# Attention scores of the 64-query step: two 64x64 matmuls, or one over the whole array with diagonal query blocks

## What is computed

```python
# attention: batch 4, heads 12, sequence 448, head dimension 64, all float32
scores = scale * q @ k.T                 # scale = 1/sqrt(64)
scores = cap * tanh(scores / cap)        # cap = 30
scores = scores - max(scores, axis=-1)
attn = exp(scores); attn = attn / (sum(attn, axis=-1) + 1e-9)
x = attn @ v                             # -> (1792, 768)
# first MLP: y = relu(x @ w_in)**2 @ w_out        (d_ff 2048)
# second: a greedy router gives each of 8 experts 224 tokens, then relu(y_e @ w1[e]) @ w2[e]
```

## Time and profile before

| | us |
|---|---|
| median of 3 runs | 1107.17 (1106.67 to 1107.28) |
| the profiled execution, its own time | 1108.04 |
| its span, first to last instruction | 1106.3 |
| attention, up to the first matmul of the MLP | 0 to 333.6 of the span |
| TensorE busy over the span | 1042.9 |
| VectorE busy | 828.0 |
| ScalarE busy | 599.2 |

### The profile page before, as it was taken

One profiled execution on the slowest core, in us unless ns is written; L12 is line 12 of the kernel. 1 busy time (PEld: TensorE's weight loads), 2 busy tenths in 40 slices (PEclk: granted clock), 3 DMA queues, 4 the chain that ended last, 5 costly groups with the idle time before them and its releaser, 6 DMA issues.

```text
span 1106.3 us, 24810 instructions
## 1 busy us (share of the span) xinstructions
PE 1042.9 (94%) x9468; PEld 846.1 (76%) x9468; DVE 828.0 (75%) x1678; ACT 599.2 (54%) x948; POOL 201.2 (18%) x322
## 2 busy tenths in 40 slices
PE   4999999899989999999999999999995999999996
PEld 1444444444449899999999999999994988888885
DVE  2989998999995965666586665566667899999971
ACT  3877777888865433323362111111326688777881
POOL 1534443444340000000000000000002132122201
PEclk9999999999999999999999999999996999999999
DMA  3561111212006000000150000002265566777401
GB/s 78 164 182 50 50 58 43 59 50 66 18 17 229 1 3 1 2 1 1 31 200 24 4 27 27 26 27 100 67 229 168 181 259 256 274 276 266 164 14 50
DMA packets 56996, 103.53 MB, mean 94 GB/s; under 512 B 6224, under 2 KB 34640, under 8 KB 56912
## 3 DMA queue, kind: packets, MB, share of 16 engines
q1 hardware_dynamic: 54352, 91.33, 24.4%
q0 software_dynamic: 2560, 11.01, 3.3%
HBM read 91.32 MB, written 11.01 MB: 93 GB/s over the span
## 4 chain that ended last, share of the span: by engine, by line
PE 83%; DVE 6%; issue 4%; ACT 4%; DMA 1%; POOL 1%; ACTq 1%; SPq 0%; DVEq 0%; POOLq 0%
PE psum L1516 20%; PE psum L1449 20%; PE psum L1650 10%; PE psum L1636 9%; PE psum L1387 6%; PE psum L1398 6%; PE psum L1407 4%; PE psum L1565 2%; DVE arena L950 2%; PE psum L1418 1%; ACT arena L652 1%; PE psum L1536 1%; PE psum L1618 1%; PE psum L1460 1%; ACT arena L647 1%
## 5 line engine op out<-in xcount | busy, mean ns | idle before, releaser
L1516 PE MATMUL psum<-arena 128*128 128x224 f16 x2304 | 232.3, 259 | 0.0
L1449 PE MATMUL psum<-arena 128*128 128x224 f16 x2304 | 223.7, 259 | 0.0
L1449 PEld LDWEIGHTS psum<-arena 128*128 128x128 f16 x2304 | 220.0, 98 | 2.9 <-issue 1.5
L1516 PEld LDWEIGHTS psum<-arena 128*128 128x128 f16 x2304 | 215.8, 98 | 1.0 <-issue 0.2
L525 POOL TENSOR_SCALAR arena<-arena 128x448 f32<-128x448 f32 x168 | 107.8, 652 | 178.8 <-DVE arena L932 178.7
L1650 PE MATMUL psum<-arena 128*112 128x384 f16 x768 | 127.1, 326 | 0.4 <-issue 0.4
L652 ACT ACTIVATE arena<-arena 128x448 f32<-128x448 f32 x168 | 125.7, 750 | 0.3 <-DVE arena L952 0.3
L1407 PEld LDWEIGHTS psum<-arena 128*112 128x112 f32 x672 | 71.7, 135 | 67.4 <-issue 53.3
L641 ACT ACTIVATE arena<-psum,arena 128x896 f32<-128x896 f32 x96 | 87.8, 914 | 63.9 <-PE psum L1387 63.6
L1650 PEld LDWEIGHTS psum<-arena 128*112 128x112 f16 x768 | 99.3, 130 | 24.8 <-issue 0.8
L1636 PE MATMUL psum<-arena 128*128 128x224 f16 x1152 | 114.5, 262 | 3.5 <-DVE arena L1300 2.0
(11 more groups left out here) (222 smaller groups left out, 1304.9 us busy)
## 6 DMA issues: line engine op xcount, KB each, us to landing
arena<-moe_w SPq DMA_DIRECT2D x16, 3072.0 KB, 12.4
arena<-moe_w_out SPq DMA_DIRECT2D x32, 384.0 KB, 3.8
arena<-moe_w_in SPq DMA_DIRECT2D x16, 384.0 KB, 5.4
arena<-q SPq DMA_DIRECT2D x24, 224.0 KB, 2.9
arena<-k SPq DMA_DIRECT2D x24, 224.0 KB, 3.1
arena<-v SPq DMA_DIRECT2D x24, 224.0 KB, 2.6
y_rows<-arena SPq DMA_DIRECT2D x16, 336.0 KB, 3.2
arena<-y_rows,arena POOLq DMA_INDIRECT x16, 4.5
```

Of the source, the lines that this page charges most:

```text
L1449: last = pe.matmul(out, w_split[:, f, z, k * 128:(k + 1) * 128], x[u % 2][:, k, :], start=(k == 0 and m == 0), stop=(k == KD - 1 and m == 2))
L1516: last = pe.matmul(out, w_split[:, k, z, m * 128:(m + 1) * 128], g[u][:, k, :], start=(k == 0 and j == 0 and (0 < u < NU - 1 or m % 2 == 0 ...
```

## The change

The fourth step's queries of both heads are laid into a 128 x 128 tile `q_mixed`: the first head's 64 queries in rows 0 to 63 and columns 0 to 63, the second's in rows 64 to 127 and columns 64 to 127, with zeros elsewhere. One matmul over all 128 rows and 128 columns then gives both heads' scores in the same places of the same bank. The zeros are written once per buffer by GpSimd at the start. ScalarE's copy of the transposed q becomes three instructions: 384 columns into `qT`, and two blocks of 64 x 64 into `q_mixed`.

```diff
+        q_mixed = [take(WIDE) for _ in range(2)]
...
-        s_pe = sem("tensor_waits_passed"); s_ym = sem("y_max"); s_sp = sem("sync_waits_passed")
+        s_pe, s_mz = sem("tensor_waits_passed"), sem("mixed_zeroed"); s_ym = sem("y_max"); s_sp = sem("sync_waits_passed")
...
             pool.memset(ones_f, 1.0).then_inc(s_one, 1)
+            for part in q_mixed:
+                pool.memset(part, 0.0).then_inc(s_mz, 1)
             pool.memset(wog_words, 0.0).then_inc(s_wz, 1)
...
                     wait(act, s_tr, 2 * (P + 2) + 1)
                     wait(act, s_S, NC * (P + 1))
-                    act.activation(qT[(i // NC) % 2], psum[:, BANK_TR, 0:S], ACT.Copy).then_inc(s_qT, 1)
+                    if is_step(P + 2, 0):
+                        act.wait_ge(s_mz, 2)
+                    act.activation(qT[(i // NC) % 2][:, 0:3 * WIDE], psum[:, BANK_TR, 0:3 * WIDE], ACT.Copy)
+                    for h in range(2):
+                        rows = slice(REST * h, REST * h + REST)
+                        last = act.activation(q_mixed[(i // NC) % 2][rows, rows], psum[rows, BANK_TR, 3 * WIDE:S], ACT.Copy)
+                    last.then_inc(s_qT, 1)
...
                         pe.sem_inc(s_pe, 1)
-                    for h in range(2):
-                        rows = slice(D * h, D * h + D)
-                        if blocks(i + 3) == 2:
-                            out, columns = psum[:, BANK_S + h, 0:S], slice(cc * WIDE, (cc + 1) * WIDE)
-                        else:
-                            out, columns = psum[REST * h:REST * h + REST, BANK_S, 0:S], slice(cc * WIDE, S)
-                        last = pe.matmul(out, qT[slot][rows, columns], kT[slot][rows], start=True, stop=True)
+                        last = pe.matmul(psum[:, BANK_S, 0:S], q_mixed[slot], kT[slot], start=True, stop=True)
+                    else:
+                        for h in range(2):
+                            rows = slice(D * h, D * h + D)
+                            last = pe.matmul(psum[:, BANK_S + h, 0:S], qT[slot][rows, cc * WIDE:(cc + 1) * WIDE], kT[slot][rows],
+                                             start=True, stop=True)
                     last.then_inc(s_S, 1)
```

## The result

The changed kernel takes 1108.88 us, the median of 20 runs (1107.12 to 1114.69), against 1107.26 for 20 runs of the kernel before beside them: a ratio of 1.0020, 95% interval 1.0011 to 1.0029. The profiled execution took 1108.81 with a span of 1107.1; before it was 1108.04 and 1106.3.

A forecast was written before the change was run, and what follows sets the result against it. It took attention to be bound by TensorE, then VectorE, then ScalarE in the splitting iterations, then TensorE and VectorE again. Terms +0.28 + 0.15 - 0.10 - 0.56 - 0.14 + 0.35 - 0.28 = -0.30 us gave 1106.9 us, range 1105.0 to 1108.8.

The forecast's parts named there:

- The rival that rested on that rule: Narrow step's weight loads not hidden under matmuls, up to +0.22 us a step: 1110.9 us, slower; chance 6%.
- the turn is not saved: Rival: float32 transposes empty the array whatever precedes them, each narrow step 0.05 us dearer: 1108.4 us; chance 18%.
- Items 3 and 4: First narrow step, about -0.10 us; then four narrow steps before VectorE is full, -0.56 us, and six later ones, nothing.
- stretch (a): Before the measuring and some pairs into it: TensorE's work back to back bounds; four narrow steps gain -0.56 us.
- stretch (b): From 99.10 to 173.81 us VectorE runs without a real hole, 12.54 us a pair; six narrow steps gain nothing.
- Item 2: Three ScalarE copies for one: +0.15 us each time, at most +0.33, covered by idle time except +0.15 at the start.
- Item 1: Two more memsets on GpSimd at the start: identity and TensorE +0.28 us later, between 0 and 0.28.
- Item 5: One narrow step behind the scale, on TensorE's chain: -0.14 us.
- Item 6: Seven pairs of the splitting iterations: transposes start sooner for nothing, scores 0.05 us later each, +0.35 us.
- stretch (c): Splitting iterations: from the narrow matmul's end the chain runs over ScalarE alone to L647; seven pairs, +0.35 us.
- Item 7: Last two iterations: two narrow steps gain 0.14 us each, -0.28 us; the last two stand before waits, nothing.
- stretch (d): Last two iterations: the chain is TensorE's again for two pairs, then VectorE's; -0.28 us.

The follow-up runs named there:

- e8: Changed kernel with the narrow step as two matmuls of all 128 rows by 64 columns each, side by side: 1105.63 us, ratio 0.9988.
- e12: The changed kernel again, no edit, in the last comparison: 1108.28 us, ratio 1.0017.
- e2: Kernel before with only ScalarE's copy of q in three parts, its matmuls unchanged: 1107.57 us, ratio 1.0010.
- e1: The kernel before, unchanged, timed once more: 1107.01 us, ratio 1.0003.
- e4: Changed kernel with the two memsets of q_mixed moved from GpSimd to VectorE: 1109.88 us, ratio 1.0024.
- e9: e8 with one ScalarE copy as before, GpSimd making the diagonal blocks by a mask multiply, its two memsets gone: 1103.91 us, ratio 0.9973.
- e11: Changed kernel with one idle matmul of 56 columns in TensorE's wait at i = 5 of the splitting iterations: 1107.65 us, ratio 1.0004.
- e7: Kernel before with ScalarE's pair copy in two halves in the splitting iterations, so TensorE waits longer: 1109.01 us, ratio 1.0021.

## Why the prediction was wrong, step by step

**The form of the new step: right in kind.** Two records, the same streaming time, the tanh later after it (74.28 - 73.22 = 1.06 us; 1.02 before, 1.07 foretold), the transposes' first load hidden. The Trainium skill, TensorE: Matmul & The Clock Gate, Part 3, has weight loads overlap only where row groups differ; here the trace disagrees, since the load of 0.13 us at 73.70 lies under a float32 pass of all 128 rows that is on record from 73.70 to 74.24. The rival that rested on that rule is out, and so is "the turn is not saved".

**Items 3 and 4, the gain a step: right in its terms, one of them too large.** The account fell by 0.73 - 0.35 = 0.38 us over the four narrow steps of stretch (a), 0.095 each, where 0.14 was booked and 0.56 in all. The rows of the second passes split it as the prediction did. From the first pass to the second it is 73.70 - 73.22 = 0.48 us for 73.11 - 72.68 = 0.43: the dearer weights, 0.05 as booked. From the second pass to the transposes it is 74.08 - 73.70 = 0.38 for 73.58 - 73.11 = 0.47: the turn, 0.09 of the 0.11. And the eight transposes take 1.04 us for 1.09: the hidden load is worth 0.05. What failed is "the transposes' first weight load (0.09 to 0.10) now hides": the load hides, but 0.09 was booked for what gave 0.05. The mark of "0.80 us or less" to the transposes compared two rows that start at different things, as said above. The Trainium skill, TensorEngine Tiling (Array Packing), Key Properties, states that a change of mode drains TensorE, and the traces agree: from a second pass to the next step it is 0.47 or 0.48 us where the tiling changes, and 0.38 where it stays, behind the narrow step after and ahead of it in e8 (73.78 - 73.41 = 0.37; the product's second pass starts at 73.41 too). After has one change fewer on the way to the transposes, e8 one fewer on the way from the product, and each is worth 0.09 to 0.10.

**Item 4, stretch (b): right.** VectorE was to hold the gain back from 99 us on, and it did. The rows in the changed kernel, 0.35, 0.35 and 0.36 us later than before:

```profile
99.45 0.17 DVE L939 TENSOR_SCALAR arena<-arena 128x2 f32<-128x2 f32 x1 [0.33 <-issue]
...
124.53 0.17 DVE L939 TENSOR_SCALAR arena<-arena 128x2 f32<-128x2 f32 x1 [0.29 <-issue]
...
174.17 0.23 DVE L961 TENSOR_SCALAR arena<-arena 128x2 f32<-128x2 f32 x1
```

A pair takes (124.53 - 99.45) / 2 = 12.54 us, as before. The tanhs ran ahead in this stretch (+0.26 to +0.09), but VectorE stayed at +0.35, and the scale, which waits for VectorE, comes 0.36 later (174.57 for 174.21). What TensorE gained in between was not kept.

**Item 2, the copies: the largest error in a price.** The blocks' durations, from the list of the instructions of L665 (shortest, median, longest in ns):

```profile
L665 ACT ACTIVATE arena<-psum x48: 203/215/220, 14.6 to 305.7; 64x64 f32<-64x64 f32 x48
```

They follow each other at about 0.22 us, not 0.10: about +0.4 a pair, where I took +0.15 and bounded it at +0.33. The upper bound's 191 ns for a block was the right kind of row, and 0.03 short of each; the 0.10 was columns plus a fixed part read off a long copy. A long copy hands over before its record ends (the 384 columns after 0.37 of 0.47 us), and a block only at its end. The group took up to 71.47 - 70.61 = 0.86 us against 0.42: 0.37 for the 384 columns, as booked, and 0.49 for the blocks. In the steady state the cover of 0.34 us held, with nothing left of it. At the start, where the prediction knew that nothing covers them, TensorE waits 0.96 us (14.20 to 15.16) for 0.69: +0.27, not +0.15; and the copies of the second pair are on its path too (25.26, idle 0.33), which the prediction had put behind a cover read off at 71 us. The account stood at +0.73 at chunk 8, and at +1.35 in e12's launch, for 0.43 - 0.10 = 0.33 booked to there; e2 has 0.9 for the copies as a whole.

**Item 1, the memsets.** The identity came 0.27 later behind an unchanged gap (8.48 for 8.49), as if the full price were paid; but the gap was 7.20, 7.64 and 7.89 us in e1, e4 and e9. This stays open.

**Item 5, behind the scale: right in sign.** -0.14 was booked, and from the scale's +0.36 to the +0.29 of chunk 52 it was -0.07. At half the clock this can't be read more finely.

**Item 6, stretch (c): wrong in sign, harmless by itself.** Not 0.05 lost a pair but 0.04 gained; which of ScalarE's waits gave it was not followed. Up to chunk 80 all terms together gave 0.00 in this pair of launches, and the prediction's own terms to there give -0.02. That is luck twice: errors that cancel (the start +0.4 more than booked, stretch (a) 0.18 and item 5 0.07 less gained, stretch (c) 0.64 better), and a launch that was 0.6 us kinder at the start than e12's.

**Item 7, stretch (d).** -0.28 was booked; the account went from +1.52 at chunk 82 to +1.51 at the first MLP matmul, so nothing came.

**The clock: the step that made the prediction wrong.** "If the dip falls elsewhere in a run, about 1 us goes or comes" treated it as noise, alike for both kernels. It isn't: a further fall costs 1.5 us (the account goes from 0.00 to 1.52 in two chunks), and its chance depends on what the change does to TensorE's idle time in stretch (c), 1.57 us grown to 1.62 at the hole ahead of the fall. The prediction wrote that there the chain is ScalarE's alone, and that the transposes start sooner "for nothing"; it didn't ask what the idle time beside it does once it grows. Nothing that it had seen said that 0.05 us would matter.

**The range.** Added up from the prediction's own bounds, its upper end is another: 1107.17 + 1.0 + 0.8 is 1109.0, not 1108.8. With its own bounds the prediction would have covered the 1108.88, and by luck, since none of these bounds stands for a further fall.

**How the 1.6 us divide.** With one idle matmul in the hole the changed kernel stands at +0.5 (e11, interval -0.5 to +1.4): its costs, mostly the start, less its gains. Two accounts agree: e11's, without a further fall, is +0.55 at chunk 92, and e12's +3.72, of which its two further falls are 3.1. The other 1.1 is the runs with further falls, as far as the medians of different comparisons can be set against each other, together with whatever else e11's hole changes. The copies alone are +0.9, and the matmul alone -0.9 in its five runs at 0.987 or more, which are not all without a fall; with intervals of about 1 us each the two can't be added up finely.

## What to carry to other kernels

Where the chain has left TensorE and its idle holes are already long, making TensorE faster lengthens them, and that can cost clock: look at the granted clock over many runs, and by stretch in the profiles, before and after; the mean clock alone hides a short fall. Ask of each rearranged copy for the price of its smallest piece, since three ScalarE copies in place of one large cost twice as much here (0.86 us for 0.42); an idle engine (here GpSimd) may do the piece for nothing. When a tiling is changed, look at the turns on both sides of the step: each change of tiling cost about 0.10 us here, and the form that shared its column halves with the matmul ahead gained more (0.15 us a pair) than the one that shared the whole array with the transposes behind (0.09), because its weights were hidden too.

## What the hardware showed that I had not expected

- Kernels with holes of at most 1.57 us in TensorE's work at one place of the loop had no run with a lower mean clock, those with a longest of 1.63 to 1.66 had 30 of 66; a fall puts TensorE at 1.2 GHz for about 3.4 us and costs about 1.5.
- A 64x64 copy from PSUM occupies ScalarE for 215 ns and hands over only then, 0.22 us after it starts, while the 384 columns ahead of it, 0.47 us long, hand over after 0.37.
- The gap on GpSimd ahead of its first select was 7.20 us (e1) to 8.88 us (e7) in the profiles, and 8.49 and 7.20 in two launches of the same kernel.
- The same kernel's TensorE was 0.6 us further at 32 us of the span in one launch than in another, because its matmuls reached full speed earlier in their order.
- From the second pass of a float32 matmul of 448 columns to the next step it took 0.47 or 0.48 us where the tiling changed and 0.38 where it stayed.
